# A gated recurrence and two wide layers: layer one for all tokens and then layer two, with the first product of each layer as seven block products

## The reference

```python
sig = 1.0 / (1.0 + np.exp(-f_logit))
f = lower_bound[None, None, :] + (1.0 - lower_bound[None, None, :]) * sig
i = 1.0 - f
for t in range(S):
    h = f[:, t] * h + i[:, t] * x[:, t]
    y[:, t] = h
...
h = x @ w_in                      # layer one, x is y from above
g = np.maximum(0.01 * h, h)
return (g @ w_out).astype(np.float32)
...
h = x @ w_in                      # layer two, x is the result of layer one
neg = h <= -beta                  # beta = 1.0
pos = h >= beta
g = np.where(pos, h, np.where(neg, 0.0, (h + beta) ** 2 / (4.0 * beta)))
return (g @ w_out).astype(np.float32)
```

## Time and profile before

| | |
|---|---|
| time, median of 3 runs | 1105.47 us (1104.82 to 1106.61) |
| span of the profiled execution, first to last instruction | 1101.2 us |
| TensorE busy | 1078.7 us, 98% |
| TensorE loading weights | 1041.4 us, 95% |
| VectorE busy | 813.1 us, 74% |
| ScalarE busy | 577.0 us, 52% |
| GpSimd busy | 42.7 us, 4% |

### The profile page before, as it was taken

How to read it: one execution, slowest core, us unless ns; L and a number is a source line. 1 busy time by engine, 2 the same in 40 slices (tenths; PEclk the granted TensorE clock), 3 DMA queues, 4 the chain that set the end, 5 groups by cost and what they waited for, 6 DMA issues and landing times.

```text
span 1101.2 us, 18595 instructions
## 1 busy us (share of the span) xinstructions
PE 1078.7 (98%) x6156; PEld 1041.4 (95%) x6156; DVE 813.1 (74%) x1542; ACT 577.0 (52%) x1210; POOL 42.7 (4%) x40
## 2 busy tenths in 40 slices
PE   4899999999999999999999999999999999999998
PEld 3899999999999999999999999999999999999997
DVE  5877777777777777777777777777777777777675
ACT  4545555555555555555555555555555555555453
POOL 5540000000000000000000000000000000000000
PEclk9999999999999999999999999999999999999999
DMA  5611020010100101010010200102001010000000
GB/s 166 172 54 30 1 44 1 14 29 14 29 0 16 27 14 29 0 29 14 14 29 0 43 0 14 29 0 43 0 14 29 14 24 0 14 0 15 1 15 13
DMA packets 105878, 27.36 MB, mean 25 GB/s; under 512 B 94272, under 2 KB 104704, under 8 KB 105856
## 3 DMA queue, kind: packets, MB, share of 16 engines
q1 hardware_dynamic: 104416, 22.36, 9.6%
q0 software_dynamic: 1440, 4.72, 1.3%
HBM read 20.84 MB, written 6.23 MB: 25 GB/s over the span
## 4 chain that ended last, share of the span: by engine, by line
PE 94%; DVE 3%; DMA 1%; SPq 1%; ACT 1%; issue 1%; DVEq 0%; ACTq 0%
PE H L657 47%; PE S L670 23%; PE S L686 16%; PE S L691 8%; SPq L254 1%; DMA bound<-in_lower_bound_dram 1%; DVE W L463 1%; DVE xT L495 0%; DMA raw<-in_moe_w_out_dram 0%; ACT W L331 0%; DVE X L510 0%; DVE H L536 0%; ACT G L389 0%; DVE G L542 0%; DVE late L528 0%
## 5 line engine op out<-in xcount | busy, mean ns | idle before, releaser
L657 PE MATMUL H<-X,W 128*128 (+2 forms) x1536 | 313.1, 339 | 13.9 <-DVE G L542 5.8
L657 PE MATMUL H<-Y,W 128*128 (+2 forms) x1536 | 309.3, 336 | 0.1
L670 PE MATMUL S<-G,W 128*128 128x384 f32 (+1 forms) x1536 | 308.3, 336 | 0.7 <-DVE Y L519 0.7
L382 ACT ACTIVATE leak<-H 128x384 f32<-128x384 f32 (+1 forms) x256 | 125.0, 488 | 321.8 <-PE H L657 311.5
L657 PEld LDWEIGHTS H<-X,W 128*128 128x128 f32 x1536 | 259.5, 189 | 27.2 <-issue 6.1
L686 PE MATMUL S<-W,G 128*128 128x512 f32 x768 | 278.1, 392 | 0.0
L670 PEld LDWEIGHTS S<-G,W 128*128 128x128 f32 x1536 | 270.8, 188 | 1.1 <-DVE G L542 1.0
L657 PEld LDWEIGHTS H<-Y,W 128*128 128x128 f32 x1536 | 270.2, 188 | 1.3 <-DVE G L564 0.8
L550 DVE SCALAR_TENSOR_TENSOR quad<-quad 128x384 f32<-128x384 f32 (+1 forms) x248 | 139.9, 564 | 118.3 <-ACT quad L396 118.2
L536 DVE TENSOR_TENSOR H<-H,leak 128x384 f32<-128x384 f32 (+1 forms) x256 | 143.6, 561 | 111.9 <-ACT leak L382 110.2
L691 PE MATMUL S<-W,G 128*128 128x256 f32 x768 | 214.9, 280 | 0.0
(11 more groups left out here) (38 smaller groups left out, 235.1 us busy)
## 6 DMA issues: line engine op xcount, KB each, us to landing
out_dram<-late SPq DMA_DIRECT2D x15, 384.0 KB, 2.4
stage_f<-in_f_logit_dram SPq DMA_DIRECT2D x56, 96.0 KB, 2.8
stage_x<-in_x_dram SPq DMA_DIRECT2D x56, 96.0 KB, 2.9
late<-in_moe_w_in_dram POOLq DMA_DIRECT2D x8, 256.0 KB, 3.2
late<-in_moe_w_out_dram POOLq DMA_DIRECT2D x8, 256.0 KB, 4.4
raw<-in_moe_w_in_dram SPq DMA_DIRECT2D x7, 256.0 KB, 4.2
raw<-in_moe_w_out_dram SPq DMA_DIRECT2D x7, 256.0 KB, 4.2
stage_f<-in_f_logit_dram SPq DMA_DIRECT2D x1, 384.0 KB, 3.4
```

Source lines behind the costliest of these rows:

```text
L382: nc.scalar.activation(leak[:, 0:n], h1_bank(i, c)[:, 0:n], ACT.Copy, scale=0.01).then_inc(s_leak, 1)
L657: last = nc.tensor.matmul(bank[:, 0:n], w_in(W, a, c, k), V[:, parity(tile), b, k, 0:n], start=(k == 0 and (a, b) == PARTS[0]), stop=(k == ...
L670: last = nc.tensor.matmul(S1[:, d, 0:n], w_out(W1, a, c)[:, d * P:(d + 1) * P], G1[:, c % RING, b, 0:n], start=(c == 0 and (a, b) == PARTS ...
```

## The change

Two things are done.

First, layer one is computed for all tokens, its result (256 x 6080) is written to DRAM (`middle`), and layer two reads it back. The tiles have 512 tokens, the first one 448: 12 tiles, twice, are 24 stages. A unit is a stage and a pair of chunks, 192 in all. W1 and W2 share one place in SBUF: GpSimd prepares W2 during layer one (from unit 14 on, spaced by waits on `s_product`) and stores it to DRAM, and SyncE loads a pair of it over W1 when the last tile of layer one is through with that pair.

Second, `up`. For a pair of chunks and a tile it is a product of 2x2 blocks by 2x2 blocks: two halves of the inputs, two chunks, and the tokens in two halves of 256. It is done in seven block products, with eight sums of blocks made beforehand: four of weights by GpSimd (`weight_sums`), four of inputs by VectorE (`input_sums_first`, `input_sums_second`). A product is three matmuls of 256 columns. Some of the sums behind the products are made by TensorE, which adds a further product onto a bank: ScalarE copies bank A out after the first product, D after the third, A after the fourth and after the seventh (`keep_products`), and VectorE then makes the hidden features H in SBUF with two adds of 512 columns. The bends work on 1024 columns of H: Prelu on ScalarE in layer one; a clip (VectorE), a square (ScalarE) and a max with a product (VectorE) in layer two. `down_features` is 12 matmuls of 512 columns, `down_tokens` 24 of 256. A down follows its up two units later. Nothing in the program is a loop any more.

The lower bound is read as two rows and turned by TensorE. `take` copies the finished banks S of a stage to SBUF, once per stage, behind the high copy of its unit.

```diff
-TILE = 384
-TILES = -(-TOKENS // TILE)
-LAST = TOKENS - (TILES - 1) * TILE
-CHUNKS = HIDDEN // P
+TILE = 512
+FIRST = 448
+SIZES = [FIRST] + [TILE] * ((TOKENS - FIRST) // TILE)
+TILES = len(SIZES)
+STARTS = [sum(SIZES[:t]) for t in range(TILES)]
+HALF = TILE // 2
-UNITS = TILES * CHUNKS
-RING = 4
...
+PAIRS = HIDDEN // (2 * P)
+STAGES = 2 * TILES
+UNITS = STAGES * PAIRS
+SECOND = TILES * PAIRS
+HI, LO = 0, 1
+LAG = 2
+G_RING = 3
+H_RING = 2
...
+            def keep_products(u):
+                n = size(u // PAIRS)
+                act.wait_ge(s_product, PRODUCTS * u + 1)
+                nc.scalar.activation(keep[:, KEEP_M1, 0:n // 2], U[:, BANK_A, 0:n // 2], ACT.Copy).then_inc(s_kept, 1)
+                act.wait_ge(s_product, PRODUCTS * u + 3)
+                nc.scalar.activation(keep[:, KEEP_M5, 0:n // 2], U[:, BANK_D, 0:n // 2], ACT.Copy).then_inc(s_kept, 1)
+                act.wait_ge(s_product, PRODUCTS * u + 4)
+                nc.scalar.activation(keep[:, KEEP_U2, 0:n // 2], U[:, BANK_A, 0:n // 2], ACT.Copy).then_inc(s_kept, 1)
+                act.wait_ge(s_product, PRODUCTS * u + 7)
+                nc.scalar.activation(keep[:, KEEP_U3, 0:n // 2], U[:, BANK_A, 0:n // 2], ACT.Copy).then_inc(s_kept, 1)
+            def leaky(u):
+                n = size(u // PAIRS)
+                h = H[:, u % H_RING, 0:2 * n]
+                act.wait_ge(s_sum, 2 * u + 2)
+                nc.scalar.activation(h, h, ACT.Prelu, alpha=0.01).then_inc(s_full, 1)
+            def bend(u):
+                n = size(u // PAIRS)
+                q = square[:, 0:2 * n]
+                act.wait_ge(s_clip, u - SECOND + 1)
+                nc.scalar.activation(q, q, ACT.Square, bias=half[:, 0:1], scale=0.5).then_inc(s_square, 1)
+            def g_high(u):
+                n = size(u // PAIRS)
+                act.wait_ge(s_full, u + 1)
+                if u >= G_RING:
+                    act.wait_ge(s_down, u - G_RING + 1)
...
+            for u in range(UNITS + LAG + 1):
+                stage, j = u // PAIRS, u % PAIRS
+                if u < UNITS:
+                    keep_products(u)
+                if 0 < u < PAIRS - 1:
+                    weights_high(u + 1)
+                ahead = (u + EARLY) // PAIRS
+                step = (u + EARLY) % PAIRS
+                first_steps = ahead == 1 and u == 0
+                if ahead < TILES and (step == 1 or first_steps):
+                    for k in range(KH):
+                        sigmoid(ahead, k)
+                if ahead < TILES and (step == 2 or first_steps):
+                    for k in range(KH):
+                        gate(ahead, k)
+                if ahead < STAGES and step == 5 and ahead > 0:
+                    high_single(ahead)
+                if ahead < STAGES and step == 6 and ahead > 0:
+                    high_sums(ahead)
+                if u < SECOND:
+                    leaky(u)
+                    g_high(u)
+                else:
+                    if u > SECOND and u - 1 < UNITS:
+                        g_high(u - 1)
+                    if u < UNITS:
+                        bend(u)
+                if u >= PAIRS + LAG and j == LAG % PAIRS:
+                    take(stage - 1)
...
+            def add_second_chunk(u):
+                n = size(u // PAIRS)
+                if u >= H_RING:
+                    dve.wait_ge(s_g, u - H_RING + 1)
+                dve.wait_ge(s_product, PRODUCTS * u + 6)
+                dve.wait_ge(s_kept, 4 * u + 3)
+                nc.vector.tensor_tensor(H[:, u % H_RING, n:2 * n].rearrange("p (a n) -> p a n", a=2),
+                                        halves(U, BANK_D, BANK_B + 1, n), halves(keep, KEEP_U2, KEEP_M1 + 1, n),
+                                        ALU.add).then_inc(s_sum, 1)
+            def add_first_chunk(u):
+                n = size(u // PAIRS)
+                dve.wait_ge(s_product, PRODUCTS * u + 7)
+                dve.wait_ge(s_kept, 4 * u + 4)
+                nc.vector.tensor_tensor(H[:, u % H_RING, 0:n].rearrange("p (a n) -> p a n", a=2),
+                                        halves(U, BANK_A, BANK_C + 1, n), halves(keep, KEEP_M5, KEEP_U3 + 1, n),
+                                        ALU.add).then_inc(s_sum, 1)
+            def clip(u):
+                n = size(u // PAIRS)
+                dve.wait_ge(s_sum, 2 * u + 2)
+                nc.vector.tensor_scalar(square[:, 0:2 * n], H[:, u % H_RING, 0:2 * n], -1.0, 1.0,
+                                        ALU.max, ALU.min).then_inc(s_clip, 1)
+            def quadratic(u):
+                n = size(u // PAIRS)
+                h = H[:, u % H_RING, 0:2 * n]
+                dve.wait_ge(s_square, u - SECOND + 1)
+                nc.vector.scalar_tensor_tensor(out=h, in0=h, scalar=1.0, in1=square[:, 0:2 * n],
+                                               op0=ALU.max, op1=ALU.mult).then_inc(s_full, 1)
...
+            def product(u, bank, a, b, fresh):
+                stage, j = u // PAIRS, u % PAIRS
+                w = size(stage) // 2
+                wa = slice((a - 1) * P, a * P)
+                vb = slice((b - 1) * w, b * w)
+                nc.tensor.matmul(U[:, bank, 0:w], W_up[:, j, HI, wa], VF[:, stage % 2, HI, vb],
+                                 start=fresh, stop=False, skip_group_check=True)
+                nc.tensor.matmul(U[:, bank, 0:w], W_up[:, j, HI, wa], VF[:, stage % 2, LO, vb],
+                                 start=False, stop=False, skip_group_check=True)
+                nc.tensor.matmul(U[:, bank, 0:w], W_up[:, j, LO, wa], VF[:, stage % 2, HI, vb],
+                                 start=False, stop=True, skip_group_check=True).then_inc(s_product, 1)
+            def up(u):
+                stage, j = u // PAIRS, u % PAIRS
+                if stage == 0:
+                    pe.wait_ge(s_w_up, j + 1)
+                if stage == TILES:
+                    pe.wait_ge(s_w2_up[j], 16)
+                if j == 0:
+                    pe.wait_ge(s_low, 2 * stage + 1)
+                if u > 0:
+                    pe.wait_ge(s_sum, 2 * u)
+                product(u, BANK_A, A11, B11, True)
+                product(u, BANK_B, A12, B21, True)
+                if j == 0:
+                    pe.wait_ge(s_low, 2 * stage + 2)
+                product(u, BANK_D, S1, T1, True)
+                pe.wait_ge(s_kept, 4 * u + 1)
+                product(u, BANK_A, S2, T2, False)
+                product(u, BANK_C, A22, T4, True)
+                pe.wait_ge(s_kept, 4 * u + 2)
+                product(u, BANK_D, S4, B22, False)
+                pe.wait_ge(s_kept, 4 * u + 3)
+                product(u, BANK_A, S3, T3, False)
...
+            pe.wait_ge(s_bound, 1)
+            for u in range(UNITS + LAG):
+                if u < UNITS:
+                    up(u)
+                if u >= LAG:
+                    down(u - LAG)
```

927 lines of the change are left out of this document (442 added, 485 removed).

## The result

The changed kernel takes 1110.9 us (median of 5 runs, 1110.1 to 1113.3), the kernel before 1105.5 us beside it (1103.3 to 1107.5): a ratio of 1.0057, 95% interval 1.0040 to 1.0075. It is slower by a little more than half a per cent. Forecast were 1099.4 us, so the time lies in the range, 11.5 us above the forecast, and on the other side of no change: a gain was forecast and a small loss came.

A forecast was written before the change was run, and what follows sets the result against it. TensorE's own instructions were taken to bound the kernel. Start to unit 8 (69 us), layer one, layer two and a 13 us tail summed to 1095.1 us; plus 4.3 around the span, forecast 1099.4, range 1068 to 1132.

The forecast's parts named there:

- so the price goes by columns: TensorE's matmuls: time goes by columns alone, 0.456 ns each, so 145,920 fewer columns save 66.5 us.
- Rival (3): TensorE: weight loads bound successive 256-column matmuls, at 0.123 us 38 us less covered waits, giving 1125 to 1135; chance 0.09.
- more than 0.12 apart: Sign of being wrong: starts of 256-column matmuls on TensorE over 0.12 us apart without a wait.
- Unit 8: Start of the first full tile, after weight loads, sums and slow first units: at about 69 us.
- Layer one behind it: Layer one after its first tile: 88 units of 5.22 us, 459.4, plus 16 and 19 us of waits.
- Layer two and the end: Units 503.5 us, plus 10 and 8 of waits, less 2.8 for the down counted at the end, plus tail 13.
- the 4.3 of the kernel before: Median time over profiled span in the kernel before, 4.3 us, added to the forecast span.
- 69 already holds 32 us of idle time: First tile: argument against a slower start, since its forecast length already included 32 us of TensorE idle time.
- rival (4): The first tile and GpSimd's collisions with VectorE cost 20 us more, giving 1119; chance 0.10.
- ScalarE's deadline inside each up: Fourth and seventh products wait for ScalarE's copies of bank A; layer one loses 0.18 us a unit, 16 us.
- rival (2): Layer two's clip on VectorE runs at the two-input rate, 1.23 us, adding 30 us for 1130; chance 0.13.
- The 0.10 a unit "even where ScalarE is free": Fourth and seventh products of each up start 0.05 us late each; 19 us over 192 units, 10 in layer two.

The follow-up runs named there:

- e2: Separate kernel of seven matmul streams only, by width: 0.2267 us a turn at 512 columns, 0.1733 at 384, 0.1200 at 256; the alternating 512/256 pair 0.3467.
- e3: Changed kernel plus 48 unread identity matmuls filling TensorE's waits before and among the first units: 1109.2 us, ratio 1.0043 to the kernel before.
- e6: Changed kernel with GpSimd computing only the first 8 columns of its five results a pair in layer one's weights: 1105.8 us, ratio 0.9996 to the kernel before.

## Why the prediction was wrong

**The step that failed: "0.24 and 0.11, the pair 0.35 for 768 columns, so the price goes by columns."** What the earlier trace rows show fits two laws almost alike, since both have 384 columns a matmul on average: 0.456 ns a column and nothing for the matmul (175.1 ns at 384), or 0.4167 a column and 13.3 ns a matmul (173.3). The change takes 145,920 columns away and adds 1344 matmuls (6144 to 7488). By the first law that saves 66.5 us. By the second it is 145,920 x 0.4167 = 60.8, less 1344 x 13.3 = 17.9, less 1.7 for the floor of the 224-column ones: 41.2. I had overstated what the change is worth on TensorE by 25 us, and dismissed the cost per matmul because one start-to-start distance was 0.117. Of the 25, 15.3 are in the forecast, as units of the changed kernel that were priced too short. The other 10 are in the price of the kernel before, which the forecast does not use. There the second law is not exact either: a steady step of 24 matmuls takes 4.208 us and not 4.16, and no run shows what the 0.05 is.

Rival (3) had the place, matmuls of 256 in succession, and gave it 9%; its reason, the weight load, is not what sets 256 columns (e2), and its size, 0.123, was not met either. The sign that I had set, starts "more than 0.12 apart", would not have shown the error: they came 0.120 apart, and that was enough.

**The same by the terms of the sum.** Unit 8: 69 forecast, 75.7 measured, +6.7. Layer one behind it: 494.4 and 495.3, +0.9. Layer two and the end: 531.7 and 538.9, +7.2. Together, before rounding, they are the 14.7 by which the span (1109.8) passed the 1095.1. The time passed its forecast by only 11.5, for the median of the changed kernel is 1.1 us above the profiled span, and I had taken over the 4.3 of the kernel before. In slots, which are the turns of the matmuls without any wait, layers one and two are larger by 1.8 and 13.5 (5.24 for 5.22 and 5.40 for 5.27 a full unit, 0.26 in each of eight units of 448 tokens in layer two), and the waits, with the end, smaller by 0.9 and 6.4. Layer two has 45 narrow matmuls in a unit and layer one 21, so the error showed in layer two alone. With the right slots the same sum gives 1114.7 us, slower: the sign hung on this step.

**Start.** "69 already holds 32 us of idle time" was not enough. The first unit starts at 18.5 for 17, the first two take 16.6 for 14 (unit 2 starts at 35.16), the six after them 6.75 each for 6.3. What rival (4) named, GpSimd in VectorE's way and slow first matmuls, was there, and a third of its 20 us came. The slow matmuls are 2 of the 6.7 (e3). Part of GpSimd's 6 us (e6) I had counted in the 6.3, so what the rest of the 6.7 is stays open.

**What was right.** The mechanism of the waits: ScalarE's deadline inside each up, the fourth product released by the copy of the first, and its size in layer one (45.02 for "about 45"; 0.20 us of waits in an ordinary unit for 0.18, and 1.5 a tile for 1.75 from the sigmoids, gates and copies; Prelu 1.058 for 1.056). The rows of the products' first matmuls, in their two shapes, are below with what they waited for. The clip takes 0.694 for 0.69, so rival (2) was out. The rule that the Trainium skill (VectorE: DVE Perf Modes, The perf-mode tier table) has on it is borne out. Groups by shape of the kernel after:

```profile
L691 PE MATMUL U<-VF,W_up 128*128 128x256 f32 x1232 | 364.2, 296 | 18.8 <-ACT keep L384 18.6
...
L691 PE MATMUL U<-VF,W_up 128*128 128x224 f32 x112 | 36.4, 325 | 20.9 <-DVE VF L550 8.7 <-ACT keep L384 5.7 <-DVE W_up L566 5.2
```

The 0.10 a unit "even where ScalarE is free" was too much in layer two: its units take 5.42 us for 5.40 of turns. By the forecast's own sum the wider turns explain most of this: the copy is ready at 1.10, and the fourth product's turn is at 9 x 0.12 = 1.08 and not 1.05. Also right, but not priced: I had found that ScalarE's order was what made layer one late, and took the order as given. Moving one instruction a unit on each of two engines was worth 24 us, more than the whole forecast margin.

**Where the gain went.** In slots: 1057.3 us before, 1016.1 after, 41.2 saved. Outside slots: 43.9 us of the span before, 93.7 after, 49.8 more. By the same count 42.5 of the 93.7 lie ahead of unit 8, 34.8 in the rest of layer one and 16.4 in layer two and the end. The forecast had 94 outside slots too (53 us of waits and 41 at start and end). That this total came out is in part luck: the start was 6.7 too short and the waits of the layers 7.3 too long.

## What to carry to other kernels

Before pricing narrower matmuls, find two widths that do not share an average, or time a stream of the new width alone: a cost per instruction and a cost per column cannot be told apart from one mix, and a start-to-start distance between unlike neighbours is no price. An algorithm that saves multiplications by adding sums and partial results pays only where the engines for these have slack: choose it layer by layer, and keep it out of the first tile, where its preparation is on the path. When one engine's queue holds both long work and a short copy with a deadline, try the order of that queue first; it costs nothing and moved more here than the algorithm.
